# Entry of a causal-attention stage: v and router products moved ahead of q and k, and K copied by GpSimd before every scaling

## The reference

```
logits = x @ w_gate                       # 4 experts
topk = two largest logits; w = exp(sel - max) / sum
for e in range(4):
    q = x @ wq[e];  k = x @ wk[e];  v = x @ wv[e]
    scores = scale * (q @ k.T), causal mask, row maximum taken off
    a = exp(scores) / sum
    out += (e in topk) * w[e] * (a @ v @ wo[e])
```

## Time and profile before

| | |
|---|---|
| median of three runs | 614.58 us |
| the profiled execution, its own time | 614.5 us |
| its span, first to last instruction | 612.7 us |
| PE busy in the span | 569.0 us (93%) |
| DVE, ACT, POOL busy | 361.6, 330.4, 266.6 us |
| mean granted TensorE clock | 0.993 |

### The profile page before, as it was taken

One profiled execution on the slowest core, in us unless ns is written; L12 is line 12 of the kernel. 1 busy time (PEld: TensorE's weight loads), 2 busy tenths in 40 slices (PEclk: granted clock), 3 DMA queues, 4 the chain that ended last, 5 costly groups with the idle time before them and its releaser, 6 DMA issues.

```text
span 612.7 us, 12176 instructions
## 1 busy us (share of the span) xinstructions
PE 569.0 (93%) x4456; PEld 486.1 (79%) x4456; DVE 361.6 (59%) x1239; ACT 330.4 (54%) x971; POOL 266.6 (44%) x453
## 2 busy tenths in 40 slices
PE   3897979998999999999999999999999999999896
PEld 1676878597876779998876679999786688999784
DVE  4988442257668773247767873236766883225763
ACT  2877422145668763234667773234666864324663
POOL 5667133024644453343653453352673353242521
PEclk9999989999999999999999999999999999999998
DMA  8903622000000042020000024020000000000010
GB/s 226 263 3 90 169 70 73 6 1 1 36 27 19 2 109 48 1 78 1 35 16 30 2 63 94 1 78 1 19 27 35 2 2 1 1 1 1 1 44 35
DMA packets 29743, 26.23 MB, mean 43 GB/s; under 512 B 5810, under 2 KB 22194, under 8 KB 29684
## 3 DMA queue, kind: packets, MB, share of 16 engines
q1 hardware_dynamic: 29684, 25.46, 14.8%
HBM read 20.74 MB, written 4.72 MB: 42 GB/s over the span
## 4 chain that ended last, share of the span: by engine, by line
PE 65%; DVE 17%; ACT 8%; issue 4%; POOL 4%; DMA 1%; SPq 1%; DVEq 0%; POOLq 0%; ACTq 0%
PE bank L1062 16%; PE bank L1064 15%; PE bank L1063 15%; PE bank L1088 7%; PE bank L1052 6%; PE bank L1073 3%; DVE pt_lo L826 3%; POOL p L511 2%; ACT pt_hi L580 2%; DVE ring L764 2%; DVE neg L909 2%; PE bank L1233 2%; ACT ring L555 2%; PE bank L1234 2%; ACT x_hi L585 1%
## 5 line engine op out<-in xcount | busy, mean ns | idle before, releaser
L1062 PE MATMUL bank<-pt_hi,vv 128*64 128x128 f32 (+1 forms) x528 | 106.4, 234 | 11.4 <-DVE x_lo L833 8.2
L425 POOL TENSOR_SCALAR ring<-ring,r 128x256 f32<-128x256 f32 (+2 forms) x160 | 74.2, 476 | 94.6 <-DVE r L776 94.5
L826 DVE TENSOR_TENSOR pt_lo<-bank,pt_hi 128x512 fp32r<-128x512 f32 (+5 forms) x176 | 84.2, 494 | 44.7 <-ACT pt_hi L580 43.7
L1064 PE MATMUL bank<-pt_hi,vv 128*64 128x128 f32 (+1 forms) x528 | 100.9, 223 | 0.0
L1063 PE MATMUL bank<-pt_lo,vv 128*64 128x128 f32 (+1 forms) x528 | 100.9, 223 | 0.0
L580 ACT CAST pt_hi<-bank 128x512 fp32r<-128x512 f32 (+5 forms) x176 | 72.9, 433 | 48.0 <-PE bank L1088 46.3
L1062 PEld LDWEIGHTS bank<-pt_hi,vv 128*64 128x64 f32 x528 | 71.5, 135 | 25.9 <-issue 11.2
L555 ACT ACTIVATE ring<-ring,neg 128x256 f32<-128x256 f32 (+2 forms) x160 | 75.1, 473 | 19.0 <-DVE neg L764 19.0
L1052 PE MATMUL bank<-kz,q 128*128 128x512 f32 (+2 forms) x160 | 73.1, 546 | 9.4 <-DMA kz<-kT 9.4
L1063 PEld LDWEIGHTS bank<-pt_lo,vv 128*64 128x64 f32 x528 | 71.7, 136 | 9.2 <-issue 2.9
L511 POOL TENSOR_SCALAR p<-p,r,wgt 128x128 f32<-128x128 f32 (+4 forms) x80 | 51.9, 653 | 53.1 <-DVE r L776 48.2
(11 more groups left out here) (132 smaller groups left out, 1527.5 us busy)
## 6 DMA issues: line engine op xcount, KB each, us to landing
q<-qT SPq DMA_DIRECT2D x16, 256.0 KB, 4.0
kz<-kT SPq DMA_DIRECT2D x32, 128.0 KB, 4.2
v_raw<-v SPq DMA_DIRECT2D x16, 256.0 KB, 3.6
out<-o_sb SPq DMA_DIRECT2D x16, 256.0 KB, 2.0
w_in_raw<-w_in SPq DMA_DIRECT2D x2, 1024.0 KB, 8.5
w_cat_raw<-wcat SPq DMA_DIRECT2D x1, 1544.0 KB, 7.1
w_spatial_raw<-wsT SPq DMA_DIRECT2D x1, 1152.0 KB, 11.3
w_outT_raw<-woT SPq DMA_DIRECT2D x1, 1024.0 KB, 5.2
```

Source lines behind the costliest of these rows:

```text
L425: last = nc.gpsimd.tensor_scalar(p, p, r1[0:r, i % 2, h:h + 1], 0.0, ALU.mult, ALU.add)
L826: last = nc.vector.tensor_tensor(pt_lo[0:r, g % 2, c0:c1], bank[0:r, 2 + g % 2, c0:c1], pt_hi[0:r, g % 2, c0:c1].bitcast(F32), ALU.subtract)
L1062: nc.tensor.matmul(to, hi_l, hi_r, start=first, stop=False)
L1064: return nc.tensor.matmul(to, lo_l, hi_r, start=False, stop=last)
```

## The change

Four edits in the entry, and one in the fold:
- PE: all five v products lead, then qk 0 to 4, scores 0 to 3, qk 5, qk 6, scores 4 and 5, then transpose 0 as before.
- ACT and DVE: the high and low parts follow the same order. `top2_a` stands behind the last `low_v3`, and `top2_b` between `low_qk(0)` and `low_qk(1)`. The maxima 0 to 3 stand behind `low_qk(4)`.
- POOL: it clears `p3` first, then makes all eight K copies, then `scale3` 0, 1 and 2.
- The fold makes the columns for v and logits (388 wide) before those for q and k (384 wide).

```diff
-FOLD = [(t, 0, CUT) for t in range(KT)] + [(t, CUT, CW) for t in range(KT)]
+FOLD = [(t, CUT, CW) for t in range(KT)] + [(t, 0, CUT) for t in range(KT)]
 # GpSimd
                 pool.wait_ge(s2_gl, 8 * (b + 1))
-                for j in range(2):
+                nc.gpsimd.memset(p3[:, 2:6, P:S], 0.0).then_inc(s_pz, 1)
+                pool.wait_ge(s_pz, b + 1)
+                for j in range(3):
                     double_k(j, False)
                     double_k(j, True)
-                nc.gpsimd.memset(p3[:, 2:6, P:S], 0.0).then_inc(s_pz, 1)
-                pool.wait_ge(s_pz, b + 1)
-                double_k(2, False)
+                double_k(3, False)
+                double_k(3, True)
...
                 scale3(0)
                 scale3(1)
-                pool.wait_ge(s3_sd, NG3 * b + 2)
-                double_k(2, True)
-                double_k(3, False)
                 scale3(2)
-                pool.wait_ge(s3_sd, NG3 * b + 3)
-                double_k(3, True)
 # ScalarE
-                for i in range(4):
+                for t in range(NT):
+                    high_v3(t)
+                high_qk(0)
+                act.wait_ge(s3_ch, 6 * b + 1)
+                nc.scalar.activation(lexp[:], wsel[:], ACT.Exp).then_inc(s3_le, 1)
+                for i in range(1, 5):
                     high_qk(i)
-                high_v3(0)
                 act.wait_ge(s_pz, b + 1)
                 exp3(0)
                 exp3(1)
-                high_v3(1)
+                high_qk(5)
                 exp3(2)
                 exp3(3)
-                high_v3(2)
+                high_qk(6)
                 exp3(4)
                 exp3(5)
-                high_v3(3)
-                high_v3(4)
-                act.wait_ge(s3_ch, 6 * b + 1)
-                nc.scalar.activation(lexp[:], wsel[:], ACT.Exp).then_inc(s3_le, 1)
-                for i in range(4, 7):
-                    high_qk(i)
 # VectorE
-                for i in range(4):
+                for t in range(NT):
+                    low_v3(t)
+                top2_a()
+                low_qk(0)
+                top2_b()
+                for i in range(1, 5):
                     low_qk(i)
-                max3(0)
-                max3(1)
-                low_v3(0)
-                max3(2)
-                max3(3)
-                low_v3(1)
+                for w in range(4):
+                    max3(w)
+                low_qk(5)
                 reciprocal3(0)
-                low_v3(2)
                 reciprocal3(1)
+                low_qk(6)
                 max3(4)
                 max3(5)
-                low_v3(3)
-                low_v3(4)
-                top2_a()
                 reciprocal3(2)
-                top2_b()
-                low_qk(4)
-                low_qk(5)
-                low_qk(6)
 # TensorE
                 pe.wait_ge(s2_gl, 8 * b + 4)
-                for i in range(4):
+                v3_product(0)
+                v3_product(1)
+                if first:
+                    pe.wait_ge(s_flo, 2 * KT)
+                pe.wait_ge(s2_gl, 8 * b + 8)
+                for t in range(2, NT):
+                    v3_product(t)
+                for i in range(5):
                     qk_product(i)
-                    if first and i == 0:
-                        pe.wait_ge(s_flo, 2 * KT)
-                pe.wait_ge(s2_gl, 8 * b + 8)
-                v3_product(0)
                 for w in range(4):
                     scores3(w)
-                v3_product(1)
-                v3_product(2)
+                qk_product(5)
+                qk_product(6)
                 scores3(4)
                 scores3(5)
-                v3_product(3)
-                v3_product(4)
-                for i in range(4, 7):
-                    qk_product(i)
```

## The result

The changed kernel takes 620.73 us (median of five runs, 619.92 to 621.16) against 614.56 us before: a ratio of 1.0096, 95% interval 1.0082 to 1.0111. That is 5.0 to 6.8 us slower. The forecast was 618.8, inside a range of 616.8 to 621.2.

The account below looks back on a forecast made before the run. PE was taken to bound the kernel, busy 20.75 of 21.80 us per entry. Four entries x 0.95 = 3.80 us plus 0.46 in the first row gave 4.26, so 614.5 became 618.8 us; range 616.8 to 621.2.

Parts of the forecast that it names:

- No wait among the v products: Five leading v products on PE: no wait between them outside the first batch row, with a margin of 0.3 us.
- the rival of waiting v products: Leading v products: without the 0.3 us margin, 3.6 us more is added, 622.4 us in all; chance 0.06.
- A new wait before qk 4 behind `top2_b`: PE before qk 4: low part 2 of q, held up behind `top2_b`, stalls it 0.77 us; start at 14.29.
- `top2_b` holds DVE for 1.65: DVE between low parts 0 and 1: `top2_b` meets one K copy and keeps its old length, 1.65 us.
- the upper bound: If the wgt multiplication met the next K copy too, lateness up to 1.5 us an entry, 621.0 us in all.
- The last K copy ahead of the scaling gives transpose 0: POOL's last K copy waits for low part 5 and delays `scale3(0)`; transpose 0 at 22.73 instead of 21.78.
- Nothing taken up behind: Behind transpose 0, scores 9 and transpose 3 move with it, so all 0.95 us an entry stays: 3.80 us.
- The first row's 0.46: First batch row: `w_o_lo` holds DVE, delays v product 0's low part and so v product 2, 0.46 us once.
- The lateness was not swallowed: Rival: waits before scores 9 and transpose 3 give back 0.86 of the 0.95 us, 615.4 us; chance 0.08.
- That rival: PE's wait before transpose 0 lowers the granted clock, 1.5 us more per entry, 624.8 us; chance 0.05.
- The faster rival: PE's own work sets transpose 0; at best 0.76 us saved per entry, 611.5 us; chance 0.05.
- The rule of the skill: A VectorE instruction with two SBUF inputs contends with a GpSimd instruction reading SBUF; the second to issue is fully blocked.

Follow-up runs that it names:

- e1_top2b_later: The changed kernel with `top2_b` on DVE moved from behind `low_qk(0)` to behind `low_qk(3)`: 618.18 us, ratio 1.0059 to the kernel before.
- e2_copies_after_weights: The changed kernel with POOL waiting for the router weights (end of `top2_b`) before its first K copy: 617.52 us, ratio 1.0050 to the kernel before.
- e3_before_copies_first: The kernel before with all eight K copies ahead of the three scalings on POOL, nothing else changed: 632.46 us, ratio 1.0282.
- e4_scales_first: The changed kernel with both j = 3 copies behind `scale3(0)` and `scale3(1)`, reciprocals 0, 1 ahead of `low_qk(5)`, exponentials 2, 3 ahead of `high_qk(5)`: 617.61 us.
- e10_w_o_later: The changed kernel with the first row's low part of w_o moved from ahead of `low_v3(0)` to behind `low_qk(3)`: one run, fold to transpose 0 43.94 us instead of 44.58.
- e7_before_copy_behind_scale: The kernel before with one edit, the high copy of j = 2 moved behind `scale3(1)` on POOL: 612.65 us, ratio 0.9972.

## Why the prediction was right, point by point

- **No wait among the v products: right.** Rows with idle there exist in the first batch row alone. The high parts follow each other every 1.45 us as PE's products do; the margin held, and the rival of waiting v products falls.
- **A new wait before qk 4 behind `top2_b`: right in place and cause (e1_top2b_later, e2_copies_after_weights), too small.** qk 4 came at 14.71 instead of 14.29. The term that was mis-sized is "`top2_b` holds DVE for 1.65": it held it for 2.11. I had taken one collision with a K copy and named a second as the upper bound, but thought of the wgt multiplication for it. It was the addition on wsum, 0.48 instead of 0.17, which is 0.31 of the 0.46. Of the rest 0.13 is the step from the weights to the low part behind them (280.58 - 280.36 = 0.22, and 285.01 - 284.92 = 0.09 before).
- **The last K copy ahead of the scaling gives transpose 0: right.** From qk 4 to transpose 0 are 291.00 - 282.51 = 8.49, and I had 8.44. e3_before_copies_first shows the same chain in the other order, with 3.01 us where 3.0 were worked out. Transpose 0 itself came at 23.20 behind the entry's first product, outside the 22.6 to 22.8 that I had named: this is the error of qk 4, carried on.
- **Nothing taken up behind: nearly right.** 0.08 to 0.10 an entry is. In e4_scales_first and e7_before_copy_behind_scale, where only one of these waits is moved, more passes from one to the other. "Scores 9 and transpose 3 with waits as before" did not hold one by one (0.68 and 0.39), but with the wait before transpose 2 their sum is 1.07 in both kernels.
- **The first row's 0.46: 0.64** (e10_w_o_later), of which 3.73 - 3.19 = 0.54 is the wait itself; no run takes the remaining 0.10 apart. I had put the start of the first entry at 123.41, from scores 0. It is 123.11: the first matmul there takes 0.59 where that of the second batch row takes 0.29, and the changed kernel has the same (0.57 and 0.28). It makes v product 2 due 0.30 later too, so the sum of 0.46 is left as it was.
- **The sum.** Per entry 1.32 (the distances) instead of 0.95, so 5.3 us, and 0.6 for the first row: 5.9. The medians differ by 6.2, and the interval is 5.0 to 6.8. Of the 1.6 us between my sum of 4.26 and the 5.9, 1.5 are the four larger entries, most of it (4 x 0.31 = 1.2) the second collision. The measured 620.73 lies 1.9 above the forecast and near the upper bound of 621.0, which I had priced for a second collision: the bound was right for its reason, though I had named the wrong instruction for it.
- **The rivals.** The lateness was not swallowed: of 1.42 at transpose 0, 1.34 is there at transpose 3 (30.16 - 28.82), and 1.32 in the distance. The wait of 1.50 left the granted clock at 1.00, as the busy time by stretch of the changed kernel shows in the wait and behind it:

```profile
290.00:291.00 1.00, 0.00 (x0) 0.03 (x1) 0.96 (x3) 0.00 (x0) 1.00 (x3) 1.00 0.00 0
291.00:292.00 1.00, 1.00 (x8) 1.00 (x9) 0.80 (x3) 0.47 (x3) 0.71 (x2) 1.00 0.00 0
```

  That rival was a real mechanism, though: with 3.61 us of idle it came, in e3_before_copies_first. The faster rival needed the chain from qk 5 to transpose 0 to be shorter than its rows; only moving instructions out of it did that (e4_scales_first), and even then a part came back as the wait for the transposed tile.

The rule of the skill held for the multiplication of lexp. The Trainium skill, page SBUF — State Buffer, section Who interferes with whom, also names `tensor_scalar` among the VectorE forms that can contend with GpSimd, when their operands meet its conditions. The trace agrees for the addition on wsum, which is such an instruction and the case that I had left out: 0.48 beside a copy, 0.17 without.

## What to carry to other kernels

Before an instruction is moved ahead on one engine, list what is behind it in the queue and which of those releases the engine that sets the time: eight copies ahead of three scalings made every scaling wait for the last k product of the entry. A small chain of vector instructions costs its length at its new place, and that length depends on what GpSimd does in the same microseconds. A wait of TensorE that is removed must be followed to the next one before it is counted: of 1.50 us removed before a transpose, 0.68 were kept.

## What the runs showed of the hardware beyond what was expected

- Some of VectorE's small instructions on SBUF wait out a GpSimd copy to its end. The product of two SBUF inputs took 0.61 to 0.64 us beside a copy and 0.18 without (six kernels with, five without). The addition of a constant to five columns took 0.48 beside and 0.17 without, and the same form on the sums of the exponentials 0.63 (from 289.26; the copy ran to 289.86).
- Others did not wait. The sum over wsel, between the two slow ones, took 0.18 at 279.41, where a copy starts too, and 0.17 in e2_copies_after_weights without one; a reciprocal of two columns took 0.17 in either case. Nor did a subtraction that reads one operand from PSUM. In e2_copies_after_weights low part 0 runs with no copy beside it, and low part 1 with one from 278.17 on:

```profile
275.90 0.92 DVE L966 TENSOR_TENSOR k_lo<-bank,k_hi 64x288 fp32r<-64x288 f32 x2 [0.24 <-ACT k_hi L661]
...
278.08 0.92 DVE L966 TENSOR_TENSOR k_lo<-bank,k_hi 64x288 fp32r<-64x288 f32 x2
```

```profile
278.17 0.66 POOL L489 CAST k_hi<-k_hi 64x576 fp32r<-64x576 f32 x1 [8.43 <-DVE wgt L939]
```

- Giving GpSimd its work later made the kernel faster (e2_copies_after_weights, e7_before_copy_behind_scale), though POOL was busy for only 6.81 of the 21.80 us of an entry.
- With 3.61 us of idle in an otherwise full TensorE, the granted clock fell to 0.50 for 3 to 5 us, once only about 1 us after TensorE had gone on (e3_before_copies_first); with 1.50 to 1.62 it stayed at 1.00 (the changed kernel, e1_top2b_later). What lies between was not tried.
